# Linear attention into a tuned two-stage MLP: the queries times the state in four 64x64 quarters of TensorE's array, with the order of some small steps changed

## The reference

```python
q_s = exp(q - max(q, -1)); q_s /= sum(q_s, -1) + 1e-9
k_s = exp(k - max(k, 2));  k_s /= sum(k_s, 2) + 1e-9
kv = einsum('bhsd,bhse->bhde', k_s, v)
x = einsum('bhsd,bhde->bhse', q_s, kv)      # -> (B*S, H*D)
x = square(relu(x @ w_in)) @ w_out          # d_ff 2048
xn = x / rms(x) * rms_g
out = (silu(xn @ w_gate) * (xn @ w_val)) @ w_out2   # d_ff 1536
```

## Time and profile before

| | us |
|---|---|
| median of three runs (1661.07 to 1661.42) | 1661.26 |
| the profiled execution's own time | 1664.02 |
| its span in the trace | 1662.3 |
| PE busy in the span | 1643.6 (99%) |
| DVE busy | 1155.2 (69%) |
| ACT busy | 616.8 (37%) |
| POOL busy | 594.0 (36%) |

### The profile page before, as it was taken

One profiled execution on the slowest core, in us unless ns is written; L12 is line 12 of the kernel. 1 busy time (PEld: TensorE's weight loads), 2 busy tenths in 40 slices (PEclk: granted clock), 3 DMA queues, 4 the chain that ended last, 5 costly groups with the idle time before them and its releaser, 6 DMA issues.

```text
span 1662.3 us, 27046 instructions
## 1 busy us (share of the span) xinstructions
PE 1643.6 (99%) x10246; PEld 1496.0 (90%) x10246; DVE 1155.2 (69%) x1753; ACT 616.8 (37%) x1056; POOL 594.0 (36%) x468
## 2 busy tenths in 40 slices
PE   7999999999999999999999999999999999999999
PEld 6999999999988888888888988988998989999999
DVE  6687667666667778887766565546555567877785
ACT  5544334333333333333334333323333334434442
POOL 3564324332102225342247644556455553000000
PEclk9999999999999999999999999999999999999999
DMA  7675555554652353444342223232321335443441
GB/s 253 200 253 174 174 167 181 182 172 140 215 172 87 122 174 117 121 122 125 108 157 71 105 92 112 89 125 87 108 94 60 111 127 175 153 152 119 149 140 52
DMA packets 151745, 230.10 MB, mean 138 GB/s; under 512 B 11840, under 2 KB 75840, under 8 KB 151616
## 3 DMA queue, kind: packets, MB, share of 16 engines
q1 hardware_dynamic: 151616, 228.38, 41.8%
HBM read 143.39 MB, written 84.93 MB: 137 GB/s over the span
## 4 chain that ended last, share of the span: by engine, by line
PE 93%; DVE 2%; POOL 2%; ACT 1%; issue 1%; SPq 0%; DMA 0%; DVEq 0%; ACTq 0%; POOLq 0%
PE bank L1876 17%; PE bank L1877 16%; PE bank L1878 16%; PE bank L1962 7%; PE bank L1963 7%; PE bank L1964 7%; PE bank L2051 5%; PE bank L2053 5%; PE bank L2052 5%; PE bank L1869 2%; PE bank L1849 1%; PE bank L1865 1%; PE bank L1897 1%; PE bank L1898 1%; PE bank L1899 1%
## 5 line engine op out<-in xcount | busy, mean ns | idle before, releaser
L1876 PE MATMUL bank<-TR,SW 128*128 128x512 f32 (+1 forms) x840 | 308.5, 367 | 0.3 <-DVE TR L1584 0.3
L1878 PE MATMUL bank<-TR,SW 128*128 128x512 f32 (+1 forms) x840 | 308.7, 368 | 0.0
L1877 PE MATMUL bank<-TR,SW 128*128 128x512 f32 (+1 forms) x840 | 308.6, 367 | 0.0
L1876 PE MATMUL bank<-TAR,SA 128*128 128x288 f32 x784 | 249.1, 318 | 0.1
L1877 PE MATMUL bank<-TAR,SA 128*128 128x288 f32 x784 | 231.2, 295 | 0.0
L1878 PE MATMUL bank<-TAR,SA 128*128 128x288 f32 x784 | 230.4, 294 | 0.0
L1962 PE MATMUL bank<-GH,W 128*128 128x512 f32 x576 | 224.2, 389 | 0.4 <-DVE GH L1489 0.4
L1964 PE MATMUL bank<-GH,W 128*128 128x512 f32 x576 | 224.2, 389 | 0.0
L1963 PE MATMUL bank<-GH,W 128*128 128x512 f32 x576 | 224.2, 389 | 0.0
L1168 ACT ACTIVATE GH<-g 128x512 fp32r<-128x512 f32 x144 | 91.1, 633 | 241.6 <-DVE g L1484 161.9
L2052 PE MATMUL bank<-SW,OA 128*128 128x256 f32 x630 | 178.3, 283 | 0.0
(11 more groups left out here) (178 smaller groups left out, 3306.8 us busy)
## 6 DMA issues: line engine op xcount, KB each, us to landing
h_scratch<-hb SPq DMA_DIRECT2D x128, 288.0 KB, 2.5
hst<-h_scratch SPq DMA_DIRECT2D x144, 256.0 KB, 2.7
araw<-a_scratch SPq DMA_DIRECT2D x18, 1536.0 KB, 6.7
a_scratch<-group SPq DMA_DIRECT2D x72, 256.0 KB, 2.0
xst<-xn_scratch SPq DMA_DIRECT2D x10, 1024.0 KB, 5.1
xn_scratch<-x SPq DMA_DIRECT2D x9, 1024.0 KB, 5.4
a_scratch<-group SPq DMA_DIRECT2D x48, 192.0 KB, 1.9
out<-ost SPq DMA_DIRECT2D x36, 256.0 KB, 2.0
```

The lines of the kernel that those rows point to most:

```text
L1876: nc.tensor.matmul(ps[:, 0:w], w_hi[:, cc], x_hi[:, c], start=opens and c == 0, stop=False, skip_group_check=True)
L1877: nc.tensor.matmul(ps[:, 0:w], w_lo[:, cc], x_hi[:, c], start=False, stop=False, skip_group_check=True)
L1878: last = nc.tensor.matmul(ps[:, 0:w], w_hi[:, cc], x_lo[:, c], start=False, stop=c == 1, skip_group_check=True)
```

## The change

**In the arithmetic of X, from batch 1 on.** The two rounds keep their names but divide the work otherwise. X0 is now head 0 of the pair and X1 head 1. Each has two matmuls instead of one: the 64x64 block of its head in `bd` is the weights, and each half of the tokens (288) is moved through it. The first half goes to PSUM partitions 0 to 63, the second to 64 to 127. Rows of the array are given by the head, columns by the half of the tokens, so the four matmuls of X0 and X1 use four different quarters. ACT reads each round in two instructions of 64 partitions instead of one of 128. Batch 0 is as before.

**In the order.** X1 moves from one step behind X0 to right behind it (and its read with the read of X0). KM, its read and the exponential stand one step later in every unit from batch 1 on. In unit 1 of batches 2 to 7, kmax, KM and its read stand three steps earlier than that rule gives: KM was right behind X0 of unit 0 and is now two steps ahead of it. All waits follow the new order.

```diff
-UNIT_PE = [("KM", -3), ("Q0", 0), ("Q1", 1), ("KV", 2), ("X0", 6), ("X1", 7)]
+UNIT_PE = [("KM", -2), ("Q0", 0), ("Q1", 1), ("KV", 2), ("X0", 6), ("X1", 6)]
-UNIT_DVE = [("qmax", -10), ("qsum", -6), ("qinv", -6), ("kmax", -9), ("readKM", -2), ("readKV", 3)]
-UNIT_ACT = [("qexp", -7), ("kexp", -1), ("readQ0", 1), ("readQ1", 2), ("readX0", 7), ("readX1", 8)]
+UNIT_DVE = [("qmax", -10), ("qsum", -6), ("qinv", -6), ("kmax", -9), ("readKM", -1), ("readKV", 3)]
+UNIT_ACT = [("qexp", -7), ("kexp", 0), ("readQ0", 1), ("readQ1", 2), ("readX0", 7), ("readX1", 7)]
...
             for what, n in events:
+                if (b > 1 and c == 1) and what in ("kmax", "KM", "readKM"):
+                    n -= 3
                 table.setdefault(max(0, base + n), []).append((what, b, c))
...
+                        for t in range(2):
+                            last = nc.scalar.activation(xa[half * D:(half + 1) * D, c, t * TA:(t + 1) * TA],
+                                                        ps[t * D:(t + 1) * D, 0:TA], ACT.Copy)
+                        last.then_inc(taken_act, 1)
...
-                    wait_taken(pe, ROUND_NO[b, "Q1" if half else "Q0", c] - 1)
-                    last = nc.tensor.matmul(ps[:, 0:TA], m.bd, m.qT[:, half * TA:(half + 1) * TA], start=True, stop=True)
+                    wait_taken(pe, ROUND_NO[b, "Q1" if half or b else "Q0", c] - 1)
+                    if b == 0:
+                        last = nc.tensor.matmul(ps[:, 0:TA], m.bd, m.qT[:, half * TA:(half + 1) * TA], start=True, stop=True)
+                    else:
+                        head = slice(half * D, (half + 1) * D)
+                        for t in range(2):
+                            last = nc.tensor.matmul(ps[t * D:(t + 1) * D, 0:TA], m.bd[head, head],
+                                                    m.qT[head, t * TA:(t + 1) * TA], start=True, stop=True)
```

More of the change, by code:

```diff
@@ L1122, in take_round @@
                 else:
-                    if b:
+                    if b == 0:
+                        nc.scalar.activation(xa[:, c, half * TA:(half + 1) * TA], ps[:, 0:TA], ACT.Copy).then_inc(taken_act, 1)
+                    else:
                         act.wait_ge(ta_lo, split_a(b - 1, B22))
-                    nc.scalar.activation(xa[:, c, half * TA:(half + 1) * TA], ps[:, 0:TA], ACT.Copy).then_inc(taken_act, 1)
+                        for t in range(2):
+                            last = nc.scalar.activation(xa[half * D:(half + 1) * D, c, t * TA:(t + 1) * TA],
+                                                        ps[t * D:(t + 1) * D, 0:TA], ACT.Copy)
+                        last.then_inc(taken_act, 1)
             def w1_split(m):
@@ L1146, in ta_split @@
                 if i in (B11, B12, B21, B22):
-                    wait_taken(act, ROUND_NO[b, "X1" if i in (B12, B22) else "X0", 1 if i in (B11, B12) else 3] - 1)
+                    wait_taken(act, ROUND_NO[b, "X1" if i in (B12, B22) or b else "X0", 1 if i in (B11, B12) else 3] - 1)
                 else:
```

## The result

The changed kernel takes 1685.17 us (median of four runs, 1682.96 to 1686.84); the kernel before, in runs beside it, 1661.34 (1661.07 to 1661.42). The ratio is 1.0143 [1.0131, 1.0154]: slower, as forecast, but 1.2 us above the range and 8.2 above the predicted 1677.0. The profiled execution of after took 1684.57 us, with a span of 1682.9.

The account below looks back on a forecast made before the run. PE, busy for 99% of the span, was taken to bound the kernel. Terms of -2.9 + 14.2 + 3.8 + 0.6 gave +15.7 us, so 1677.0 us on the median of 1661.26, range 1670 to 1684.

Parts of the forecast that it names:

- Bound by PE, every added wait lost: First large product: PE busy in all of a 54.88 us window, so removed PE instructions save time and added waits lose it.
- Term 1: X0 and X1 together in four quarters: 0.84 us against 0.97 before, 0.13 less in 22 units, -2.9 us.
- Term 2: Unit 0 of batches 2 to 7: X1 waits for readKM on DVE, +2.24 us each, 0.8 more in batch 2, +14.2 us.
- Term 3: Unit 2 of batches 2 to 7: KV waits because readKM falls behind the h_22 additions, +0.63 us six times, +3.8 us.
- Term 4: Small effects: readQ0 and KV some 0.1 us later six times, +0.6 us; ACT's added reads and DMAs cost nothing.
- (a): Rival: X1 waits, but row halves do not overlap fully; three or four places, 1682 or 1688 us; chance 0.16.
- (b): Rival: passes of neighbouring fp32 matmuls keep strict order, five places instead of two for the X pair, 1693 us; chance 0.04.
- (c): Rival: additions over KM on DVE are not late, so X1 and KV do not wait, 1657.6 us; chance 0.07, later 0.08.
- (d): Rival: only the wait of X1 is missing and KV's stays, +0.8 us, 1662 us; chance 0.04.
- (e): Rival: the waits are there but shorter, as PE's pause lets later parts come in time, 1668 to 1673 us; chance 0.07.

Follow-up runs that it names:

- e1: Changed kernel with its new order of steps, but the X rounds as before the change (one matmul, one read each): 1681.37 us, ratio 1.0125.
- e4: Changed kernel with X rounds in quarters, but the order of steps from before the change, X0 and X1 a product apart: 1680.62 us, ratio 1.0115.
- e7b: Changed kernel with only readKM of unit 1 moved, ahead of both h_22 additions on DVE: 1672.70 us, ratio 1.0058.
- e2: Changed kernel without the special rule for unit 1 of batches 2 to 7, so kmax, KM and readKM stand three steps later: 1663.68 us, ratio 1.0015.
- e10: The kernel of e5b measured again, unchanged: 1660.06 us, ratio 0.9993.
- e5b: Changed kernel with KM, its read, kexp and X reads moved in units 0 to 2 to take away waits, quarters kept: 1659.98 us, ratio 0.9988.
- e9: e5b with unit 0's move made in batch 1 too and KM's move in batch 2 one step smaller: 1659.31 us, ratio 0.9992.
- e8b: e5b with the X pair in column halves (128 rows, 64 columns per matmul) instead of quarters: 1673.16 us, ratio 1.0062.

## Why the prediction was right in direction and 8.2 us short

**Bound by PE, every added wait lost: right.** The added waits and rounds come to 15.9 us between the first and last KV, against a sum of 15.7. That the two are so near is in part luck: terms 2 and 3 came out 1.2 smaller than forecast, and a smaller saving of the pair, term 4 and single waits that the sum did not have made up for it.

**Term 1, the pair at 0.84: right.** It measures 0.843, against 0.964 for the two old rounds a step apart (2 x 0.482) and 0.968 for them as a pair (e1): 0.12 to 0.125 less, where 0.13 was said. The 0.35 that was read off KV's round is the 0.347 of e4.

**Term 2, X1 behind readKM, 2.24 each: right in mechanism and size.** X1's wait is 2.35 over a pair of 0.843, so the two rounds cost 3.20 where they cost 0.97 before: +2.23. In batch 2 they cost 4.01 against 1.67, +2.34, where I had 0.8 more: before, X0 was itself late there, and what I added had to be set against that. The term is 13.5 instead of 14.2.

**Term 3, KV of unit 2, 0.63: right, 0.555 measured,** 3.3 instead of 3.8. **Term 4:** Q1 of unit 0 waits 0.12, and Q1 of unit 2 waits 0.07, which I had not seen; 1.1 instead of 0.6. ACT's added reads cost nothing. In batches 1 and 2 the later KM also brings single waits of Q1 (0.64, ahead of the first KV) and of KV (0.55).

**The step that failed** is the price of the idle in term 2. "PE idles nearly 1.9 of it" stands there (1.67 was measured), and the sum charges it at its own length, as if PE went on afterwards at the speed of the earlier trace rows. It did not: in three of six batches it went on at half clock, for 3.4 to 6.8 us. The sum had no term for the clock, neither as a cost nor as a rival. It measures 6.2 us in the profiled execution and, by e7b, 7.4 of the 8.2 at the median; the other 0.8 is the sum's own.

How much of that the wait explains: with the wait cut from 1.67 to 0.85 and the quarters kept, all four runs have a whole clock (e7b). In this stage only the traces with X1's long wait show a fall (after and e1; those of e2 to e10 show none). So the long wait is what the falls hang on here, and the quarters alone do not bring them (e4, e5b, e7b). Whether the quarters add to them when the wait is there is open (e1). Outside this stage the clock falls now and then: in batch 0 of before and of e1, and once, 3.4 us, near 1390 us in e9. Why it comes in batches 4, 5 and 7 and not in 2, 3 and 6, whose waits are as long or longer, no run here tells; the mean clocks say that it differs from run to run.

**The rivals.** (a) and (b) are out: eight records take two places, 0.843. By the Trainium skill (TensorE: Matmul & The Clock Gate, Part 3, "The mechanism") matmuls start and end in program order. If that held for the passes of neighbouring fp32 matmuls too, as (b) had it, the pair would have taken five places, 1.57; here it measures 0.843. (c) and (d) are out by PE's waits: DVE's readKM ended at 164.21, when X0 had long been over, and e2 shows what (d) would have given, 1663.7. (e) came true only in e7b, where I made it so. The 1685.2 lies between the 1682 and the 1688 of (a), but for another reason, so its nearness to them supports nothing. Beside the rivals stands a slip: (c) has a chance of 0.07 in its own paragraph and 0.08 in the count that follows.

## What to carry to other kernels

When small rounds take turns in a few buffers, a changed order changes whose reading each one waits for: look up, for every round, which read frees its buffer and what stands ahead of it on the reading engine. Price a new wait of TensorE in a dense stream twice, by its length and by what the clock may cost behind it: here 1.67 us of idle cost up to 3.0 us more, 0.85 us nothing. A smaller division of the array pays only if enough matmuls stand next to each other to share one change of the division: 0.12 gained by four together, 0.35 lost by two.

## What the runs showed of the hardware

The clock was the surprise. In a stream that kept PE busy for all of 54.88 us, idle of 1.67 us was followed by the half level (1.2 instead of 2.4 GHz) at three of five places in one run, and idle of 2.49 us was not; in e1 it followed the idle of 2.61 us and one of five of 1.84 us. Behind the 0.82 to 0.85 us of e7b, five times in its trace, it never came, nor behind its one idle of 1.63 us, and the mean clock of each of its four runs is 1.00. What the half level cost is 3.0 us for 6.8 at it and 1.5 to 1.6 for 3.4, since a large matmul went from 0.133 to 0.24 us.

Four quarters of the array work truly at once, also for the two passes of fp32: eight records of 288 columns take as long as two (0.486) plus 0.35, and only 0.014 more than four records in two quarters (e4). Four matmuls in column halves take four places (1.316). The change of the division there and back costs 0.35, whether to 64x64 (0.347 in e4), to 128x64 (e8b, 1.316 - 0.972 = 0.344) or for KV.
